# Identity matmuls in TensorE's waits, an earlier kv and a third bank for q's turns in a fused attention kernel

## What is computed

```python
q_s = softmax(q, axis=-1)           # over a head's 64 columns
k_s = softmax(k, axis=2)            # over the 576 rows of the sequence
kv = einsum('bhsd,bhse->bhde', k_s, v)
x = einsum('bhsd,bhde->bhse', q_s, kv)      # heads side by side: (8, 576, 512)
h = gelu(x @ w_in)                  # 512 -> 1024, halves u and v
v_n = layernorm(v) * g_ln
x1 = x + (u * (w_sg @ v_n + b_sg)) @ w_out
h2 = relu(x1 @ w_in2)               # 512 -> 1024
out = (h2 * sigmoid(conv3(h2))) @ w_out2
```

## Time and profile before

| | |
|---|---|
| median of 3 runs | 946.67 us (946.52 to 947.38) |
| profiled execution | 948.56 us |
| its span, first to last instruction | 946.8 us |
| mean granted TensorE clock | 0.991 |
| busy: PE, DVE, ACT, POOL | 98%, 64%, 40%, 38% |
| instructions | 14688 |

### The profile page before, as it was taken

The page is one execution under the profiler, slowest core; times in us unless marked ns, Lnnn a source line. Parts: engine busy times, 40 slices in busy tenths (PEclk is TensorE's granted clock), DMA queues, the critical chain, the costliest instruction groups (busy, mean ns, idle before and its releaser), DMA issues.

```text
span 946.8 us, 14688 instructions
## 1 busy us (share of the span) xinstructions
PE 923.9 (98%) x5980; PEld 864.1 (91%) x5980; DVE 601.5 (64%) x943; ACT 374.9 (40%) x564; POOL 361.9 (38%) x230
## 2 busy tenths in 40 slices
PE   6899899999999999999999998999999999999998
PEld 5799799899999998999999997999998989999987
DVE  6667666657746666576355797866667666667660
ACT  3561433524524335245234254533434333434331
POOL 4985545446426444464204133322222222232320
PEclk8899999999999999999999999999999999999999
DMA  8815425134061151330412302020202020200001
GB/s 256 251 48 178 134 51 193 37 100 158 12 200 56 45 194 41 99 109 12 134 64 82 111 13 73 12 84 23 73 23 73 23 73 23 84 23 22 25 23 55
DMA packets 50482, 77.84 MB, mean 82 GB/s; under 512 B 4336, under 2 KB 22768, under 8 KB 49520
## 3 DMA queue, kind: packets, MB, share of 16 engines
q1 hardware_dynamic: 45808, 67.48, 22.6%
q10 hardware_dynamic: 4608, 9.44, 2.7%
HBM read 56.97 MB, written 18.89 MB: 80 GB/s over the span
## 4 chain that ended last, share of the span: by engine, by line
PE 89%; DVE 6%; DMA 2%; issue 1%; ACT 1%; POOL 1%; SPq 0%; ACTq 0%; DVEq 0%; POOLq 0%
PE psum L452 51%; PE psum L444 29%; PE psum L510 3%; PE psum L593 2%; PE psum L486 2%; PE psum L545 1%; DMA plain_arena<-in_q 1%; DVE plain_arena L1322 1%; DVE split_arena L1304 1%; DMA x_dram<-plain_arena 1%; DVE plain_arena L1133 0%; DVE plain_arena L1246 0%; DVE split_arena L1462 0%; DVE plain_arena L1320 0%; DVE plain_arena L1215 0%
## 5 line engine op out<-in xcount | busy, mean ns | idle before, releaser
L452 PE MATMUL psum<-split_arena 128*128 128x288 f32 x4032 | 559.0, 297 | 6.0 <-DVE split_arena L1201 2.9
L452 PEld LDWEIGHTS psum<-split_arena 128*128 128x128 f32 x4032 | 545.9, 189 | 12.6 <-DVE split_arena L1201 3.2
L444 PE MATMUL psum<-split_arena 128*128 128x512 f32 x1248 | 298.3, 393 | 2.7 <-DVE split_arena L1462 2.6
L444 PEld LDWEIGHTS psum<-split_arena 128*128 128x128 f32 x1248 | 232.2, 189 | 49.8 <-DVE split_arena L1462 3.5
L1614 POOL TENSOR_TENSOR plain_arena<-plain_arena 128x576 f32<-128x576 f32 x64 | 107.4, 1678 | 281.6 <-ACT plain_arena L915 281.6
L1325 DVE SCALAR_TENSOR_TENSOR plain_arena<-plain_arena 128x576 f32<-128x576 f32 x64 | 96.2, 1503 | 2.2
L1320 DVE TENSOR_SCALAR plain_arena<-plain_arena 128x576 f32<-128x576 f32 x64 | 36.0, 563 | 90.1 <-ACT plain_arena L909 90.1
L1555 POOL TENSOR_TENSOR plain_arena<-plain_arena 128x576 f32<-128x576 f32 x32 | 46.5, 1453 | 110.6 <-DVE plain_arena L1259 110.6
L909 ACT ACTIVATE plain_arena<-psum 128x576 f32<-128x576 f32 x64 | 41.6, 650 | 105.4 <-PE psum L452 74.4
L915 ACT ACTIVATE plain_arena<-plain_arena 128x576 f32<-128x576 f32 x64 | 43.7, 683 | 43.5 <-DVE split_arena L1462 40.4
L1462 DVE TENSOR_TENSOR split_arena<-plain_arena,split_arena 128x576 fp32r<-128x576 f32 x64 | 53.2, 832 | 10.9 <-ACT split_arena L921 10.0
(11 more groups left out here) (80 smaller groups left out, 787.0 us busy)
## 6 DMA issues: line engine op xcount, KB each, us to landing
x_dram<-plain_arena ACTq DMA_DIRECT2D x32, 288.0 KB, 2.1
plain_arena<-x_dram SPq DMA_DIRECT2D x8, 1152.0 KB, 5.7
out_rows<-plain_arena SPq DMA_DIRECT2D x36, 256.0 KB, 2.0
plain_arena<-in_v SPq DMA_DIRECT2D x32, 256.0 KB, 3.3
plain_arena<-in_kT SPq DMA_DIRECT2D x7, 1152.0 KB, 8.0
plain_arena<-in_q SPq DMA_DIRECT2D x7, 1024.0 KB, 5.7
plain_arena<-in_k SPq DMA_DIRECT2D x7, 1024.0 KB, 5.6
plain_arena<-in_w_in SPq DMA_DIRECT2D x8, 512.0 KB, 5.8
```

The costliest lines, as they stand in the source:

```text
L444: mm = e.matmul(out, stat[s], mov[m], start=first and n == 0, stop=last and n == 2, skip_group_check=True)
L452: mm = e.matmul(out[:, h, 0:NH], stat[s], mov[m][:, h * NH:(h + 1) * NH], start=first and n == 0, stop=last and n == 2, skip_group_check=True)
```

## The change

`keep_clock(n)` issues n float32 matmuls of the 128x128 identity with itself into the first 128 columns of bank 3, which nothing reads. `first_attention` on PE calls it six times: 10 matmuls after the kmax spread, 3 after the kv pieces, 3 after q's turns 0 and 1, 4 after turn 2, 3 after turn 3, 4 after turn 4. All five kv pieces come ahead of q's first turn; before, the fifth stood between turns 1 and 2. In batch 0 q's third tile is turned into bank 2, so turn 2 waits for no `lo_q`, and turns 3 and 4 for those of tiles 0 and 1. On ACT `hi_kv` goes to the front, `hi_q` of tile 1 ahead of `hi_w(1)`, `hi_w(2)` behind all of q's copies. On DVE `finish_kv` goes ahead of the second `sum_q`, and `lo_kv` ahead of the second `lo_q`. The other batches keep their order.

```diff
--- before.py
+++ after.py
@@ -156,8 +156,10 @@
         psum_row = psum[:, :, :].rearrange("p a n -> p (a n)")
         k_raw = [psum_row[:, 2 * d * BANK:2 * d * BANK + T] for d in range(DT)]
         kmax_bank = psum[:, 1, :]
+        idle_bank = psum[:, 3, 0:P]
         qsum_first = psum[:, 0, 0:NJ * NT]
         q_banks = [psum[:, 7, :], psum[:, 6, :]]
+        q_banks_first = [psum[:, i, :] for i in (7, 6, 2, 7, 6)]
         x_banks, x_banks_odd = psum[:, 6:8, :], psum[:, 2:4, :]
         y_banks = [psum[:, 4 + i, :] for i in range(4)]
 
@@ -270,6 +272,10 @@
         def o_set(b, d):
 
             return (o_sets_last if isinstance(b, int) and b == B - 1 else o_sets)[d]
+
+        def q_bank(b, j):
+
+            return q_banks_first[j] if first(b) else q_banks[j % 2]
 
         def x_place(b, d):
 
@@ -475,15 +481,18 @@
                 mm.then_inc(k_spread, 1)
 
             def turn_q(b, j):
-                if j > 1:
+                if first(b):
+                    if j > 2:
+                        e.wait_ge(q_lo, j - 2)
+                elif j > 1:
                     e.wait_ge(q_lo, b * NJ + j - 1)
-                elif not first(b):
+                else:
                     e.wait_ge(x_lo, b * DT)
                 if j == NJ - 1:
                     e.wait_ge(pad_set, 2)
                 e.wait_ge(q_norm, b * NU + j // 2 + 1)
                 for d in range(DT):
-                    mm = e.transpose(q_banks[j % 2][:, d * P:(d + 1) * P], qs[:, j, d * P:(d + 1) * P], ident)
+                    mm = e.transpose(q_bank(b, j)[:, d * P:(d + 1) * P], qs[:, j, d * P:(d + 1) * P], ident)
                 mm.then_inc(q_turned, 1)
 
             def kv_piece(b, j):
@@ -636,19 +645,29 @@
                                      [x2[h][:, d, :] for h in (0, 1)], d == 0, d == DT - 1)
                 mm.then_inc(h_done, 1)
 
+            def keep_clock(n):
+
+                for _ in range(n):
+                    e.matmul(idle_bank, ident, ident, start=True, stop=True, skip_group_check=True)
+
             def first_attention():
 
                 for u in range(NU):
                     turn_raw_k(u)
                 spread_first_kmax()
-                for j in range(NJ - 1):
+                keep_clock(10)
+                for j in range(NJ):
                     kv_piece(0, j)
+                keep_clock(3)
                 turn_q(0, 0)
                 turn_q(0, 1)
-                kv_piece(0, NJ - 1)
+                keep_clock(3)
                 turn_q(0, 2)
+                keep_clock(4)
                 turn_q(0, 3)
+                keep_clock(3)
                 turn_q(0, 4)
+                keep_clock(4)
                 x_piece(0, 0)
                 x_piece(0, 1)
 
@@ -801,7 +820,7 @@
                 if j == 0 and not first(b):
                     e.wait_ge(x_done, b * DT)
                 e.activation(qT[0][:, :, j * P:j * P + rows],
-                             q_banks[j % 2].rearrange("p (a b) -> p a b", a=DT)[:, :, 0:rows],
+                             q_bank(b, j).rearrange("p (a b) -> p a b", a=DT)[:, :, 0:rows],
                              ACT.Identity).then_inc(q_hi, 1)
 
             def hi_kv(b):
@@ -936,15 +955,15 @@
                 exp_q(0, 0)
                 exp_q(0, 1)
                 exp_q(0, 2)
+                hi_kv(0)
                 hi_w(0)
                 hi_q(0, 0)
+                hi_q(0, 1)
                 hi_w(1)
-                hi_q(0, 1)
-                hi_kv(0)
                 hi_q(0, 2)
-                hi_w(2)
                 hi_q(0, 3)
                 hi_q(0, 4)
+                hi_w(2)
                 hi_w(3)
                 hi_x(0, 0)
                 hi_late(W_SG, w_sg_raw, w_sg_hi[2], 2)
@@ -1172,7 +1191,7 @@
                 rows = P if j < NJ - 1 else TAIL
                 e.wait_ge(q_hi, b * NJ + j + 1)
                 cols = slice(j * P, j * P + rows)
-                e.tensor_tensor(qT[1][:, :, cols], q_banks[j % 2].rearrange("p (a b) -> p a b", a=DT)[:, :, 0:rows],
+                e.tensor_tensor(qT[1][:, :, cols], q_bank(b, j).rearrange("p (a b) -> p a b", a=DT)[:, :, 0:rows],
                                 f32(qT[0][:, :, cols]), ALU.subtract).then_inc(q_lo, 1)
 
             def finish_kv(b):
@@ -1335,12 +1354,12 @@
                 max_q(0, 1)
                 max_q(0, 2)
                 sum_q(0, 0)
+                finish_kv(0)
                 sum_q(0, 1)
                 sum_q(0, 2)
                 lo_q(0, 0)
-                finish_kv(0)
+                lo_kv(0)
                 lo_q(0, 1)
-                lo_kv(0)
                 lo_q(0, 2)
                 lo_q(0, 3)
                 lo_q(0, 4)
```

## The result

Twenty runs of each kernel: **951.46 us** after (947.79 to 955.68), 947.35 before (945.44 to 950.51). The ratio is **1.0038, 95% interval 1.0026 to 1.0051**: slower by 0.4%, where 946.0 us was forecast. The ratios are formed from all runs; the quotient of two medians can lie 0.001 from them. One single run of all, of f2_after_pad, was in a slower state of the chip (1301.01 us at a granted clock of 0.656) and counts in no ratio. The profiled execution of after took 953.56 us, its span 951.8, 5.0 more than before's 946.8.

What follows compares the result with a forecast made beforehand. TensorE, busy 98%, was taken as the bound, so only its waits or half-clock stretches give time back. Of 1.8 us won at the v stream's start, 0.7 survives: 946.67 to 946.0 us, own range 945.6 to 946.4, 8-in-10 range 944.0 to 948.0.

Steps and rivals of the forecast that it cites:

- What is late next: Wait for vn's moved tail before 64.47: sub_k of batch 1 starts 0.65 us earlier, PE's restart about 0.7 us earlier.
- so the shift stays: Behind 64.47 us: PE's next wait, ending at 95.03, follows PE's own turns, so the gain is kept.
- C: Opening: fillers stand in the path at half clock, so slower, 947.8 to 948.6 us; chance 0.14.
- Part 1: Ten identity matmuls after the kmax spread: 20 passes, 2.2 us inside a wait, cost nothing; clock holds past 13.7 us.
- Part 2: All five kv pieces first: 40 passes from 14.95 end at about 19.6 us; no gain in itself.
- Part 3: kv's normalisation before q's second and third sums on DVE: q's second sum 1.15 us later, third turn at 24.6, not 23.62.
- Parts 4 and 5: q's tail with its own bank, then x piece at 28.75 and v matmuls at 31.55 us; 1.8 us together at v's start.
- The sum: Whole kernel: a gain of 0.7 us, from a median of 946.67 to 946.0 us.
- Rival A: The whole 1.8 us arrives, kmax landing before 47.2 us: 945.0 us; chance 0.18.
- Rival B: Half-clock dip after 98 us changes too: gone, 944.3 us (0.15), or longer, 947.4 us (0.05); chance 0.20.
- Rival D: The clock falls at 27.3 us as before although filled; gain 0.4 at most, hidden: 946.3 to 946.7 us; chance 0.06.

Runs made afterwards that it cites:

- f2_after_pad: The changed kernel plus 24 one-column matmuls in TensorE's first wait, 204 instructions more than before; 951.27 us, ratio to before 1.0024.
- c1_after: The changed kernel run once more, unaltered, beside its parts; 951.89 us, ratio to before 1.0028.
- f1_wide: The changed kernel with the fillers' columns in eight wide matmuls, 32 instructions more than before; 947.98 us, ratio to before 1.0000.
- g2_kv_late_256: The changed kernel with kv's normalisation back behind q's sums and 37 one-column matmuls, 256 instructions more than before; 945.63 us, ratio to before 0.9986.
- g1: The changed kernel plus 37 one-column matmuls in TensorE's first wait, 256 instructions more than before; 947.46 us, ratio to before 1.0003.
- f3_before_pad: The kernel before plus 27 one-column matmuls ahead of everything, 108 instructions more; 950.75 us, ratio to before 1.0023.
- h1: The kernel before plus 64 one-column matmuls in TensorE's first wait, 256 instructions more; 946.65 us, ratio to before 0.9993.
- g4: f4 with batch 1's first sub_k moved on POOL behind the copies and its third behind scale_q; 948.22 us, ratio to before 1.0002.
- e3: The changed kernel with kv's normalisation put back behind q's sums on DVE, all 27 fillers kept; 950.45 us, ratio to before 1.0014.
- g3: f4 plus 56 one-column matmuls, 256 instructions more than before; 946.13 us, ratio to before 0.9983.
- e2_fill_only: The kernel before, order and banks unchanged, with the same 27 identity matmuls added; 951.59 us, ratio to before 1.0024.
- f4: The changed kernel with kv's normalisation back behind q's sums and eight wide fillers, 32 instructions more than before; 946.76 us, ratio to before 0.9990.
- h2_no_fill_108: The changed kernel's order and bank without fillers, with 27 one-column matmuls in TensorE's first wait, 108 instructions more than before; 952.07 us, ratio to before 1.0055.

## Why the prediction was wrong

**The step that failed** is the last sentence of "What is late next": behind 64.47 nothing changes, "so the shift stays". I looked only for waits that the change touches through semaphores. What it also changes is the number of instructions ahead of each later one, and with it the moments at which blocks of instructions are fetched. The missing term: a store of 2.1 us becomes one of 4.0 to 4.6, PE waits 1.7 to 2.2, and where the clock falls behind that (four of the six profiles) the half clock adds 1.7. No step had a price for it. Worked out from before's trace it could have been seen: the transfer of 233.6 comes 108 instructions of program earlier; a transfer came every 15.4 us (218.2 to 233.6) for 256, so 108 are 6.5 us and it lands at 227.1, right in the stores of 225.66 to 229. None of the rivals had it; C had the sign, by another mechanism.

By the prediction's own steps:

- **Part 1 (fillers free, clock holds): right in c1_after**, 2.40 us for 20 passes. In after's profile it failed: the clock fell at 11.5, kv began at 15.33, or 15.79 with k's 0.46 added, against 14.95; kv still took 4.64.
- **Part 2 (40 passes in 4.6): right**, 4.64 and 4.74.
- **Part 3 (turn 2 at 24.6): right, and the harm is real.** c1_after 24.11 with k landed 0.73 earlier, so 24.84; f1_wide 24.54 with 0.29, 24.83. With kv's normalisation late it is 23.25 (g2 below). PE waits 1.52 there in c1_after and 0.21 in g2_kv_late_256.
- **Parts 4 and 5 (x piece 28.75, v 31.55): right.** f1_wide: 28.60 and 31.27, with 0.29 added 28.89 and 31.56. c1_after with 0.73 added: 28.95 and 31.63.
- **What is late next (`sub_k` at 48.15, tail at 63.8, wait 1.6): the wait is right, the size was met in one profile.** PE waits 1.58 to 1.60 in all five profiles of the changed order with fillers. f1_wide with its 0.29 added has 48.15 and 63.78, the forecast to the digit. But with k's landing set off in the same way the tail is at 63.97 in f2, 64.28 in c1, 64.58 in g1 and 66.42 in after, and in before's own order with pads at 63.35 (f3) and 64.15 (h1), against before's 64.47. So the 0.7 lies within what moves without any change, and the exact hit of f1_wide is partly luck.
- **The sum (0.7 us gained): not shown by the medians, nor excluded.** Without the transfer after is at 1.0000 (f1) and 1.0003 (g1); g1's interval, -0.8 to +1.3 us, just holds -0.7. f1's profile is 0.94 us ahead of before's from 110 to 500 us, 0.29 of it k's landing, and loses 1.3 at 575, where the clock fell as it did not in before's. The base was off too: the sum starts from the median of three runs, 946.67, where twenty gave 947.35.
- **Rival A fell**: `sub_k` began at 47.86 to 50.34 in the five profiles of the changed order with fillers, never before 47.2.
- **Rival B: the dip changes, both ways.** Behind 98 us the half clock is absent in six of the other fifteen profiles, as long as in before in seven (in g1 from 96.1) and 6.8 us long in two (c1, g4). From 98 to 110 us a profile gains up to 3.5 us on before's or loses up to 1.3, more than the whole forecast. See below.
- **Rival C: met in one of two profiles of after**, with +1.29 us at 224 (1.1 was worked out); it is not what made the median.
- **Rival D fell**: the clock held in c1_after.

The rule of the Trainium skill (TensorE: Matmul & The Clock Gate, Part 4) that transposes don't count for the clock is not borne out by c1_after. There k's 20 transposes are PE's only work ahead of 8.89:

```profile
4.68 3.69 PE L471 MATMUL psum<-plain_arena 128*128 128x128 f32 x20 [4.68 <-DMA plain_arena<-in_k]
```

In before the same 20 took 4.80. In c1_after they begin 0.21 us apart up to 7.27 and 0.11 from 7.44, and the trace's record of the clock begins at 7.38, with 1.00: the clock rose to full behind transposes alone. Whether q's turns alone would hold it no run shows, since in c1_after fillers lie between them.

**What gains.** Undo Part 3 and take the transfer off the stores. Timeline of PE in g2_kv_late_256, and its stretches at 98 and 102.5 (columns as in the earlier trace rows):

```profile
23.25 0.66 PE L495 MATMUL psum<-plain_arena 128*128 128x128 f32 x4 [0.21 <-POOL plain_arena L1535]
...
28.42 1.82 PE L458 MATMUL psum<-split_arena 128*128 128x288 f32 x12 [0.68 <-DVE split_arena L1196]
30.99 3.02 PE L450 MATMUL psum<-split_arena 128*128 128x512 f32 x12 [0.74 <-DVE split_arena L1222]
```

```profile
98.00:102.00 4.00, 2.87 (x15) 2.55 (x16) 3.93 (x8) 1.60 (x2) 1.59 (x1) 1.00 0.57 138
102.50:106.00 3.50, 3.50 (x19) 3.01 (x18) 1.51 (x2) 2.38 (x3) 3.50 (x3) 1.00 0.51 153
```

Its v matmuls start at 30.99, no earlier than in c1_after, so its 0.14% (945.63 us, the best of all) does not come from the opening. In its profile it comes from the stretch after 98: PE is busy 2.87 of 4.00 us, waits 1.5 us instead of the 2.9 of before, and the clock stays at 1.00 where the earlier trace rows have 0.50. That was rival B's first half. At the addition near 224, e3, g2, g3 and f2 are 3.8 to 4.3 us ahead of before, the eleven others between 1.9 ahead and 1.3 behind (f3 and h1, with before's own order, 1.9 and 1.3 ahead).

What shortens the wait at 99 the profiles show in part. DVE's addition ahead of it waits for the first x1 store of batch 0. before, then g2_kv_late_256:

```profile
99.92 0.76 DVE L1290 TENSOR_TENSOR plain_arena<-psum,split_arena 128x576 f32<-128x576 f32 x1 [2.81 <-DMA x_dram<-plain_arena]
```

```profile
97.65 0.76 DVE L1311 TENSOR_TENSOR plain_arena<-psum,split_arena 128x576 f32<-128x576 f32 x1 [1.36 <-DMA x_dram<-plain_arena]
```

That store took 4.89 us in before and 3.45 in g2, and in fifteen of the sixteen profiles PE's wait is its time less 1.9 to 2.0 us (in g1 the clock had fallen just before). It runs beside a load of v. It took 3.0 to 3.6 us in f2, g2 and g3, where v had landed by 95.8 and no q8 packet came in between; 3.8 to 5.0 in e2, e3 and f3, where v had landed by 95.9 but a q8 packet left at 94.3 to 95.9; and 4.0 to 5.1 in the others, where v landed at 96.4 or later. This is read from one profile of each; no run tests it, and what moves v's load stays **open**. kv late is not enough for it: f4 and g4 have it and not the short wait, and f2 has the short wait with kv early.

That kv late is a gain is likely, but not shown by any single ratio: g2 against g1 is 0.9986 against 1.0003, f4 against f1 0.9990 against 1.0000. The mean times of runs of the same rounds all differ the same way: e3 less c1 -1.1 us (95% interval 1.8 either way), f4 less f1 -1.1 (1.1), g2 and g3 less g1 -1.2 (0.9). Through which wait it would come isn't shown.

## What to carry to other kernels

Before adding or removing a hundred instructions on an engine, even free ones in front of everything, list when its instruction transfers fall and which transfers of data with no slack lie within the shift; in a kernel that is bound by TensorE at 98%, two microseconds of a late store come back as nearly four if the clock falls behind them. Test an inserted idle-filler against its bare count (same number, one column each) and against a whole block of 256, before you believe what its work did. That an instruction transfer meets a store is not yet a loss: ask whether the next step waits for that store. And prefer few wide instructions for filling: the same columns cost 32 instructions here instead of 108.

## What the runs showed of the hardware that I had not expected

- A 16 KB instruction transfer of TensorE, under way for 0.9 to 1.9 us beside the first x1 stores of batch 2, went with a doubling of a 288 KB store's time: 4.0 to 4.6 us in the six profiles with it, 2.1 in the ten without. The rate at the end of the store in after, 25 to 38 GB/s against 385, looks like one engine left at work.
- A matmul of one column costs 0.03 us a pass (54 in 1.49 us), so padding is almost free in time; it is not free in place.
- A wait of 2.0 us cost little more than itself in h2_no_fill_108 (2.1), and another 1.7 in after, c1_after, e2_fill_only and f3_before_pad, whose clock was half afterwards. Near 575 us PE waits 1.97 us in all 16 profiles; the clock was half behind it in seven of them, and these lost 1.3 us there.
- The same kernel, run again, lost a half-clock stretch or not: g2_kv_late_256 took 944.5 us at a mean clock of 1.0 and 948.6 at 0.994. Over the fifteen kernels the mean clock goes with about six tenths of the variance of one kernel's runs.
- The start of the same addition in an unchanged order moved by up to 1.9 us at 224 us, with only one-column matmuls put in front (f3, h1): one profile is too few to read a microsecond at the end from.
